# Seven products of half blocks in place of eight, in three blocks of a fused attention and expert kernel

## The chip, the cores and the metric

The kernel runs as one program on one core of a Trainium2 chip. The metric is the device time of one execution in microseconds (us). Lower is better.

## The reference

An attention with a pooled part and a local part gives x. A dense layer with an ELU in the middle works on x (this is layer 1), and a layer of four gated experts works on its result. All data are float32.

```python
# attention, 2 batches x 8 heads x 576 tokens x 64: pooled by 4, plus a band of +-3 tokens
x = attention(q, k, v)                      # 1152 tokens x 512
h = x @ w_in                                # 512 x 2048
g = np.where(h > 0.0, h, np.exp(np.minimum(h, 0.0)) - 1.0)
y = g @ w_out                               # 2048 x 512
for e in range(4):                          # p: normalised domain_probs
    out += p[:, e:e + 1] * (np.maximum(y @ w1[e], 0.0) @ w2[e])   # 512 x 1024 x 512
```

## The kernel before

**Splitting.** Every large product is made of three matmuls: an operand is split into a high part, which ScalarE casts, and a low part, which GpSimd (weights) or VectorE (activations) gets by a subtraction, and high by high, low by high and high by low are summed in PSUM. Each x, h, wa (up weights) and wb (down weights) thus exists as `_hi` and `_lo`.

**Layer 1** is cut into 8 blocks: 4 blocks of 512 hidden columns for the first batch of 576 tokens (blocks 0 to 3, mixed with the attention of the second batch) and the same 4 for the second batch (blocks 4 to 7). A block has 16 groups (`group1`), each of 12 matmuls of 128 x 128 by 288 tokens into one PSUM bank of 4 (`MOE_BANKS`). Groups 0 to 7 are the up projection (4 column tiles by 2 token halves), groups 8 to 15 the down projection. Behind an up group comes a chain: ScalarE takes relu(-h) (L782) and its exponential (L785), VectorE forms the ELU in PSUM (L1057), ScalarE casts `h_hi` (L791), VectorE subtracts `h_lo` (L1063). Behind a down group VectorE copies (block 4, L1078) or adds (L1080) the bank into `y_acc`, and its semaphore `y_added` frees the bank.

**Layer 2** is cut into 16 steps (`step2`): 8 halves of 512 hidden columns (two of each expert), each for the tokens of step 0 (2 x 256) and of step 1 (2 x 320). Its up projection is a two by two block product in Strassen's form (Winograd's variant): 7 products instead of 8. For this the weights need three sums of quarters (`s_raw`, L1343 to L1348 on GpSimd, then `s_hi` on ScalarE, L822, and `s_lo` on GpSimd, L1352), the tokens three sums of quarters (`add_y`: step 0 on GpSimd, L1316 to L1324, step 1 on VectorE, L1161 to L1169), and VectorE adds products to one another (`u2_sum` L1102, `w_sum` L1108, C22 L1114, C12 L1120, C21 L1125).

**Order.** It is written out by hand: each engine runs its own list, and semaphores tie them. The lists that matter are in `block`'s functions: `group1` on every engine, on GpSimd the sequence behind its loop (`split_wb`, `add_y(0)`, `split_wa`, `split_y(0)`, a memset of `o_acc` in block 5), on VectorE the four gate instructions ahead of block 5 (L1254 to L1260). SyncE loads wa and wb of the next block when both parts of the present one exist.

Of the kernel before, what the change touches and what calls it, by code (L numbers as in the profile page):

```python
# [54 lines left out]

QF = FB // 2
# [8 lines left out]
T2_, T1_, T4_ = range(3)  # L65
# [36 lines left out]
def program(nc, q, k, v, w_in, w_out, probs, w1, w2, out):  # L102
# [12 lines left out]
    with ExitStack() as ctx:  # L115
# [110 lines left out]
        t_raw_ready = sem("t_raw_ready")  # L226
        qT_copied, kT_copied = sem("qT_copied"), sem("kT_copied")
# [123 lines left out]
        def _(pe):  # L351
# [202 lines left out]

            def step2(j, b):
# [27 lines left out]

                pe.wait_ge(y_lo_ready, Y_PARTS * b + 2)
# [5 lines left out]
                pe.wait_ge(s_lo_ready, 3 * j + 1)  # L590
# [14 lines left out]
                for p in range(PAIRS2):  # L605
                    pe.wait_ge(u2_ready, PAIRS2 * v + p + 1)
                    product2(bank(BANK_B, p), weights(1, 0, p), tokens(0, 1), False, False, p7_done)
                pe.wait_ge(s_lo_ready, 3 * j + 3)
                for p in range(PAIRS2):
                    pe.wait_ge(w_ready, PAIRS2 * v + p + 1)  # L610
                    product2(bank(BANK_C, p), weight_sum(S4, p), tokens(1, 1), False, True, p3_done)
                pe.wait_ge(y_lo_ready, Y_PARTS * b + 7)
                for p in range(PAIRS2):
                    pe.wait_ge(c22_ready, PAIRS2 * v + p + 1)
# [97 lines left out]
            with pe.Fori(BLOCKS1 + 1, 2 * BLOCKS1) as w:  # L712
                for g in range(GROUPS1):
                    group1(w, 1, g)
# [8 lines left out]
        def _(act):  # L723
# [83 lines left out]
            def split_first2(n):  # L807

                act.wait_ge(wa_loaded, 16 * (2 * BLOCKS1 + 1))
                act.wait_ge(group_done, groups_before1(2 * BLOCKS1 - 1) + UP1)  # L810
                split_w2(0, n)

            def split_w2(j, n):

                if n in (0, 1, 3, 4):
                    c = n if n < 2 else n - 1
                    act.wait_ge(s_raw_ready, 4 * j + 3)
                    nc.scalar.copy(wa_hi[:, c, :], wa_raw[:, c, :]).then_inc(wa_hi_ready, 1)  # L818
                else:
                    q = {2: S2, 5: S1, 6: S4}[n]  # L820
                    act.wait_ge(s_raw_ready, 4 * j + 4 if q == S4 else 4 * j + 3)
                    nc.scalar.copy(s_hi[:, q], s_raw[:, q]).then_inc(s_hi_ready, 1)  # L822

            def step2(j, b, border=False):
# [19 lines left out]
                for p in range(PAIRS2):  # L844
                    act.wait_ge(p2_done, PAIRS2 * v + p + 1)
# [6 lines left out]
                for p in range(PAIRS2):  # L852
                    act.wait_ge(c22_ready, PAIRS2 * v + p + 1)
# [6 lines left out]
                for p in range(PAIRS2):  # L860
                    act.wait_ge(c12_ready, PAIRS2 * v + p + 1)
                    hidden_hi(0, 1, p, BANK_C)
                for p in range(PAIRS2):
                    act.wait_ge(c21_ready, UNIT_CREDIT + PAIRS2 * v + p + 1)
                    hidden_hi(1, 0, p, BANK_B)

            def next_weights2(j):

                act.wait_ge(p4_done, PAIRS2 * (2 * j + 2))
                act.wait_ge(wa_loaded, 16 * (2 * BLOCKS1 + j + 2))  # L870
                for n in range(KC + 3):
                    split_w2(j + 1, n)
# [87 lines left out]
            after = {9 + n: [(split_y, 0, n)] for n in range(Y_PARTS)}  # L960
            for g in range(GROUPS1):
                group1(BLOCKS1, 1, g, after.get(g, ()))
            with act.Fori(BLOCKS1 + 1, 2 * BLOCKS1 - 1) as w:
                for g in range(GROUPS1):
                    group1(w, 1, g)
# [496 lines left out]
```

## Time and profile before

| what | value |
|---|---|
| three runs | 659.1, 659.1, 659.29 us |
| median | 659.1 us |
| profiled execution, its own time | 658.5 us |
| span in its trace, first to last instruction | 656.7 us |
| mean granted TensorE clock | 0.999 |

The span leaves 1.8 us of the profiled execution's time ahead of and behind the instructions. The profiled execution is 0.6 us shorter than the median of the runs.

### The profile page before, as it was taken

What the parts mean: (1) busy time and instruction counts of PE and PEld (TensorE: products, weight loads), DVE (VectorE), ACT (ScalarE), POOL (GpSimd) and SP (SyncE); (2) the same over time, 40 slices, a digit from 0 to 9 for tenths busy, and PEclk for the clock granted to TensorE, in tenths of its full rate; (3) what the DMA queues carried; (4) which work ended last, traced back from release to release, by engine and by line L of the source; (5) the groups of instructions that cost most, each with busy time, mean ns of one, the idle gap of its engine ahead of it and who ended that gap; (6) DMA issues with size and microseconds to landing.
All of it is one profiled execution on the core that took longest, in us unless ns stands there. A gap on an engine that the chain in (4) does not pass through costs nothing.

```text
span 656.7 us, 12912 instructions
## 1 busy us (share of the span) xinstructions
PE 647.1 (99%) x4734; PEld 597.4 (91%) x4734; DVE 321.6 (49%) x715; ACT 278.3 (42%) x759; POOL 304.5 (46%) x266
## 2 busy tenths in 40 slices
PE   8999999999999999999999999999999999999998
PEld 5788999999999999998998998899899899899986
DVE  5856454545354343475534544453464355265352
ACT  4888383838295374464224133142152152142110
POOL 4674444443399444888426336138047065160210
PEclk9999999999999999999999999999999999999999
DMA  9954434332112311301103003003011011010012
GB/s 184 246 131 110 122 83 117 87 94 73 64 65 67 127 64 64 117 12 65 65 1 129 1 0 128 0 6 122 0 64 64 0 64 64 1 64 1 1 49 96
DMA packets 51489, 46.11 MB, mean 70 GB/s; under 512 B 31616, under 2 KB 33920, under 8 KB 51456
## 3 DMA queue, kind: packets, MB, share of 16 engines
q1 hardware_dynamic: 51456, 45.67, 23.5%
q8 instruction: 21, 0.34, 0.2%
q14 instruction: 12, 0.10, 0.0%
HBM read 43.30 MB, written 2.36 MB: 70 GB/s over the span
## 4 chain that ended last, share of the span: by engine, by line
PE 90%; ACT 5%; DVE 4%; issue 1%; ACTq 0%; DVEq 0%
PE psum L474 19%; PE psum L476 19%; PE psum L475 19%; PE psum L549 9%; PE psum L551 9%; PE psum L547 9%; ACT attn L741 1%; PE psum L466 1%; DVE neg_max L1013 1%; ACT attn_p L741 1%; PE psum L397 1%; PE psum L460 1%; PE psum L421 1%; ACT sums L782 1%; PE psum L441 1%
## 5 line engine op out<-in xcount | busy, mean ns | idle before, releaser
L1302 POOL TENSOR_TENSOR wb_lo<-wb_raw,wb_hi 128x512 fp32r<-128x512 f32 x64 | 82.0, 1295 | 202.4 <-ACT wb_hi L774 202.4
L1142 DVE SCALAR_TENSOR_TENSOR o_acc<-psum,gate_now,o_acc 128x512 f32<-128x512 f32 x72 | 54.1, 751 | 126.0 <-PE psum L476 125.7
L476 PE MATMUL psum<-wb_hi,h_lo 128*128 128x512 f32 x288 | 112.3, 390 | 0.0
L475 PE MATMUL psum<-wb_lo,h_hi 128*128 128x512 f32 x288 | 112.2, 390 | 0.0
L474 PE MATMUL psum<-wb_hi,h_hi 128*128 128x512 f32 x288 | 112.0, 389 | 0.0
L831 ACT ACTIVATE h_hi<-psum 128x320 fp32r<-128x320 f32 (+1 forms) x128 | 52.5, 412 | 87.4 <-DVE psum L1114 40.4
L1302 POOL TENSOR_TENSOR wa_lo<-wa_raw,wa_hi 128x512 fp32r<-128x512 f32 x60 | 76.0, 1294 | 22.6 <-ACT wa_hi L818 14.1
L837 ACT COPY sums<-psum 128x256 f32<-128x256 f32 (+1 forms) x32 | 12.8, 400 | 156.7 <-PE psum L551 156.7
L474 PE MATMUL psum<-h_hi,wb_hi 128*128 128x288 f32 x256 | 76.8, 300 | 0.0
L476 PE MATMUL psum<-h_hi,wb_lo 128*128 128x288 f32 x256 | 75.4, 294 | 0.0
L475 PE MATMUL psum<-h_lo,wb_hi 128*128 128x288 f32 x256 | 75.3, 294 | 0.0
L474 PE MATMUL psum<-x_hi,wa_hi 128*128 128x288 f32 x232 | 70.0, 302 | 1.7 <-DVE h_lo L1063 1.2
L475 PE MATMUL psum<-x_lo,wa_hi 128*128 128x288 f32 x232 | 68.3, 295 | 0.0
L476 PE MATMUL psum<-x_hi,wa_lo 128*128 128x288 f32 x232 | 68.3, 295 | 0.0
L476 PEld LDWEIGHTS psum<-wb_hi,h_lo 128*128 128x128 f32 x288 | 54.0, 188 | 11.3
L474 PEld LDWEIGHTS psum<-wb_hi,h_hi 128*128 128x128 f32 x288 | 54.1, 188 | 10.8
L475 PEld LDWEIGHTS psum<-wb_lo,h_hi 128*128 128x128 f32 x288 | 54.0, 188 | 10.8
L1096 DVE SCALAR_TENSOR_TENSOR h_lo<-psum,h_hi 128x320 fp32r<-128x320 f32 (+1 forms) x128 | 54.9, 450 | 17.0 <-ACT h_hi L831 17.0
L551 PE MATMUL psum<-x_hi,wa_lo 128*128 128x256 f32 (+1 forms) x192 | 56.8, 296 | 0.0
L549 PE MATMUL psum<-x_lo,wa_hi 128*128 128x256 f32 (+1 forms) x192 | 56.7, 295 | 0.0
L547 PE MATMUL psum<-x_hi,wa_hi 128*128 128x256 f32 (+1 forms) x192 | 56.6, 295 | 0.0
L1057 DVE SCALAR_TENSOR_TENSOR psum<-sums,psum 128x288 f32<-128x288 f32 x64 | 29.6, 462 | 45.9 <-ACT sums L785 45.9
(163 smaller groups left out, 1529.0 us busy)
## 6 DMA issues: line engine op xcount, KB each, us to landing
wa_raw<-in_moe_w_in SPq DMA_DIRECT2D x8, 1024.0 KB, 5.7
wb_raw<-in_moe_w_out SPq DMA_DIRECT2D x8, 1024.0 KB, 5.0
wa_raw<-in_moe_w SPq DMA_DIRECT2D x8, 1024.0 KB, 4.9
wb_raw<-in_moe_w SPq DMA_DIRECT2D x8, 1024.0 KB, 5.0
out<-o_acc SPq DMA_DIRECT2D x9, 256.0 KB, 2.0
q_in<-in_q SPq DMA_DIRECT2D x10, 144.0 KB, 4.3
k_in<-in_k SPq DMA_DIRECT2D x10, 144.0 KB, 4.3
v_in<-in_v SPq DMA_DIRECT2D x5, 288.0 KB
```

The lines of the kernel that those rows point to most:

```text
L474: nc.tensor.matmul(bank_cols, w_hi(n), x_hi_(n), start=(n == 0), stop=False)
L475: nc.tensor.matmul(bank_cols, w_hi(n), x_lo_(n), start=False, stop=False)
L476: last = nc.tensor.matmul(bank_cols, w_lo(n), x_hi_(n), start=False, stop=(n == chunks - 1))
L547: nc.tensor.matmul(bank, w_op[0][:, k, :], x_op[0][:, k, :], start=(start and k == 0), stop=False, skip_group_check=True)
L549: nc.tensor.matmul(bank, w_op[0][:, k, :], x_op[1][:, k, :], start=False, stop=False, skip_group_check=True)
L551: last = nc.tensor.matmul(bank, w_op[1][:, k, :], x_op[0][:, k, :], start=False, stop=(stop and k == 1), skip_group_check=True)
L741: last = nc.scalar.activation(out[:, c, :], psum[:, bank, width * (c - c0):width * (c - c0 + 1)], ACT.Exp, bias=neg_max[:, stat:stat + 1], ...
L831: nc.scalar.activation(h_hi[:, 2 * fh + p, t0 + width * th:t0 + width * (th + 1)], psum[:, bank[p], 0:width], ACT.Relu).then_inc(h_hi_read ...
L1057: nc.vector.scalar_tensor_tensor(bank, elu_exp[:, g % 2, 0:N1], -1.0, bank, ALU.add, ALU.max).then_inc(elu_ready, 1)
L1096: nc.vector.scalar_tensor_tensor(h_lo[at], bank(banks, p), 0.0, h_hi[at].bitcast(F32), ALU.max, ALU.subtract).then_inc(h_lo_ready, 1)
L1142: nc.vector.scalar_tensor_tensor(o_acc[:, m, :], psum[:, DOWN2_BANKS[(MT * half + m) % 2], :], gate_now[:, m:m + 1], o_acc[:, m, :], ALU.m ...
L1302: nc.gpsimd.tensor_tensor(lo[:, c, :], raw[:, c, :], hi[:, c, :].bitcast(F32), ALU.subtract).then_inc(lo_ready, 1)
```

## The change

Block 4 stays in the old form. Blocks 5, 6 and 7 (`block7`, `BLOCKS7 = 3`, `FIRST7 = 5`) form their up projection of 512 columns by 576 tokens from seven products of half blocks, with 288 tokens a half, in the way of `step2`. Their down projection keeps its 96 matmuls, in another order: the four groups of the first token half first take hidden chunks 0 and 1, then 2 and 3; the other four follow whole. It uses banks 6, 7, 0, 3, 6, 7, 6, 7.

TensorE's list of the up projection and the two gates that the down projection has at its end:

```diff
+            def block7(w):
+                for p in range(PAIRS2):
+                    pe.wait_ge(y_added, y_before - 5 + p)
+                    product2(bank(BANK_A, p), weights(0, 0, p), tokens(0, 0), True, False, p1_done)
+                pe.wait_ge(s_lo_ready, 3 * v + 1)
+                for p in range(PAIRS2):
+                    product2(bank(BANK_B, p), weight_sum(S2, p), token_sum(T2_), True, False, p6_done)
...
+                    product2(bank(BANK_A, p), weights(0, 1, p), tokens(1, 0), False, True, p2_done)
...
+                    product2(bank(BANK_C, p), weight_sum(S1, p), token_sum(T1_), True, False, p5_done)
...
+                    pe.wait_ge(u2_ready, PAIRS2 * v + p + 1)
+                    product2(bank(BANK_B, p), weights(1, 0, p), tokens(0, 1), False, False, p7_done)
+                for p in range(PAIRS2):
+                    pe.wait_ge(c22_ready, PAIRS2 * v + p + 1)
+                    product2(bank(BANK_B, p), weights(1, 1, p), token_sum(T4_), False, True, p4_done)
...
+                    product2(bank(BANK_C, p), weight_sum(S4, p), tokens(1, 1), False, True, p3_done)
...
+                pe.wait_ge(h_lo_ready, h_before + 8)
+                for g in range(KC, 2 * KC):
+                    pe.wait_ge(y_added, y_before + (1, 2, 5, 6)[g - KC])
+                    for f in range(FC):
+                        down(g, f)
```

The sums of x quarters need x unsplit. The attention of the second batch therefore writes its output into the second half of `y_acc` (free until block 4's down projection) and not into `x_sum`, and VectorE forms four sums ahead of block 4's groups; T3 takes the place of the x quarter (0, 1).

```diff
+            def add_x():
+                dve.wait_ge(out_free, OUT_CREDIT + 2 * PAIRS)
+                nc.vector.tensor_tensor(xt_raw(T1_), x_quad(0, 1), x_quad(0, 0), ALU.subtract).then_inc(xt_raw_ready, 1)
+                nc.vector.tensor_tensor(xt_raw(T3_), x_quad(1, 1), x_quad(0, 1), ALU.subtract).then_inc(xt_raw_ready, 1)
...
+            add_x()
+            lows = {12: [(xt_lo, 1, T2_)], 13: [(xt_lo, 2, T1_)], 14: [(xt_lo, 3, T4_)], 15: [(xt_lo, 4, T3_)]}
```

VectorE runs something beside the `y_acc` adds of each new block (`beside(g)` behind the add of group g): in block 5 the token sums of step 0 (`add_y(0, g)`, before on GpSimd), in block 6 the gates, in block 7 the memset of `o_acc` (before on GpSimd), whose first three rows serve as `s_raw1` until then.

```diff
+                for g in range(2 * KC):
+                    dve.wait_ge(group_done, groups_before7(w) + g + 1)
+                    nc.vector.tensor_tensor(y_acc[at], psum[:, DOWN7_BANKS[g], 0:N1], y_acc[at], ALU.add).then_inc(y_added, 1)
+                    beside(g)
...
+            def clear_out(g):
+                if g == 0:
+                    dve.wait_ge(s_lo_ready, 3 * BLOCKS7)
+                    nc.vector.memset(o_acc[:], 0.0).then_inc(acc_zeroed, 1)
```

GpSimd's list behind its loop:

```diff
-            add_y(0)
-            split_wa(BLOCKS1 + 1)
-            split_y(0)
-            split_wb(BLOCKS1 + 1)
-            nc.gpsimd.memset(o_acc[:], 0.0).then_inc(acc_zeroed, 1)
...
+            add_ws(FIRST7, s_raw1)
+            split_ws(FIRST7, s_raw1)
+            split_wb(FIRST7)
+            pool.wait_ge(s_lo_ready, 3)
+            add_ws(FIRST7 + 1, s_raw1)
+            split_ws(FIRST7 + 1, s_raw1)
+            split_y(0, range(3))
+            split_wb(FIRST7 + 1)
...
+            split_ws(FIRST7 + 2, s_raw1)
+            split_y(0, range(3, Y_PARTS))
```

ScalarE copies the first product twice a block (`copy_p1`), has the same ELU chain with a buffer of its own (`elu7`), and casts the next block's weights and weight sums at the block's end (`split_ws`).

How the lists stand, at three places. VectorE at the end of block 5, before:

```order
L1063 TENSOR_TENSOR h_lo<-psum,h_hi 128x288 [waits h_hi_ready] x2
L1076 ISA
L1080 TENSOR_TENSOR y_acc<-psum,y_acc 128x288 [waits group_done]
L1076 REGISTER_ALU
L1080 TENSOR_TENSOR y_acc<-psum,y_acc 128x288 [waits group_done]
```

and in the changed kernel (L1299 is `h_lo`, L1356 the add into `y_acc`, `h_spare` the memory of the token sums):

```order
L1299 TENSOR_TENSOR h_lo<-psum,h_hi 128x288 [waits h_hi_ready] x2
L1356 TENSOR_TENSOR y_acc<-psum,y_acc 128x288 [waits group_done]
L1436 TENSOR_TENSOR h_spare<-y_acc 128x512 [waits y_added]
L1356 TENSOR_TENSOR y_acc<-psum,y_acc 128x288 [waits group_done]
L1440 TENSOR_TENSOR y_acc<-y_acc 128x2x256 [waits t_raw_ready]
L1356 TENSOR_TENSOR y_acc<-psum,y_acc 128x288 [waits group_done]
L1443 TENSOR_TENSOR h_spare<-y_acc,h_spare 128x512
L1356 TENSOR_TENSOR y_acc<-psum,y_acc 128x288 [waits group_done]
```

Between the first five adds of block 5 now stand four operations of 512 elements. At the end of block 7, VectorE in the changed kernel:

```order
L1299 TENSOR_TENSOR h_lo<-psum,h_hi 128x288 [waits h_hi_ready] x2
L1356 TENSOR_TENSOR y_acc<-psum,y_acc 128x288 [waits group_done]
L1559 MEMSET o_acc 128x4608 [waits s_lo_ready]
L1356 TENSOR_TENSOR y_acc<-psum,y_acc 128x288 [waits group_done] x7
```

The memset stands between the first add and the other seven; before, it was GpSimd's (L1422), in block 5. TensorE in the middle of a new block (the first matmul of each product; L571 is `product2`'s first line):

```order
L571 MATMUL psum<-x_hi,wa_hi 128x288 [waits u2_ready]
...
L571 MATMUL psum<-t_hi,wa_hi 128x288 [waits c22_ready]
L573 MATMUL psum<-t_lo,wa_hi 128x288
L575 MATMUL psum<-t_hi,wa_lo 128x288
```

The first row opens the second half of product 7, and the row with `c22_ready` the first half of product 4, which follows at once. In `step2` product 3 lies between the two.

## Rows read from the trace of the kernel before

**Rows 1.** the page: busy time of TensorE with its share.

```profile
PE 647.1 (99%) x4734; PEld 597.4 (91%) x4734; DVE 321.6 (49%) x715; ACT 278.3 (42%) x759; POOL 304.5 (46%) x266
```

**Rows 2.** waits of TensorE: us in total, times, longest.

```profile
PE psum L474 <- DVE h_lo L1063: 1.2, 1, 1.2
```

**Rows 3.** TensorE's timeline (start us, us, line): block 5, two steps of layer 2.

```profile
202.45 0.29 PE L474 MATMUL psum<-x_hi,wa_hi 128*128 128x288 f32 x1
...
278.77 0.28 PE L547 MATMUL psum<-x_hi,wa_hi 128*128 128x256 f32 x1
...
288.73 0.30 PE L547 MATMUL psum<-x_hi,wa_hi 128*128 128x320 f32 x1
```

**Rows 4.** timeline of VectorE in block 6: two adds into y_acc.

```profile
250.33 0.46 DVE L1080 TENSOR_TENSOR y_acc<-psum,y_acc 128x288 f32<-128x288 f32 x1 [1.14 <-PE psum L476]
251.93 0.46 DVE L1080 TENSOR_TENSOR y_acc<-psum,y_acc 128x288 f32<-128x288 f32 x1 [1.14 <-PE psum L476]
```

**Rows 5.** timeline around a wait of TensorE in block 0.

```profile
57.43 0.46 DVE L1063 TENSOR_TENSOR h_lo<-psum,h_hi 128x288 fp32r<-128x288 f32 x1 [1.39 <-ACT h_hi L791]
57.95 0.41 PE L474 MATMUL psum<-x_hi,wa_hi 128*128 128x288 f32 x1 [1.24 <-DVE h_lo L1063]
58.19 0.30 PE L475 MATMUL psum<-x_lo,wa_hi 128*128 128x288 f32 x1
```

**Rows 6.** timeline: last matmul of a product 7 in step2, C22 behind it.

```profile
285.06 0.28 PE L551 MATMUL psum<-x_hi,wa_lo 128*128 128x256 f32 x1
...
285.38 0.43 DVE L1114 TENSOR_TENSOR psum<-psum,sums 128x256 f32<-128x256 f32 x1 [0.28 <-PE psum L551]
```

**Rows 7.** timeline of the ELU chain and the casts in block 7.

```profile
263.05 0.41 ACT L782 ACTIVATE sums<-psum 128x288 f32<-128x288 f32 x1 [0.40 <-PE psum L476]
263.97 0.46 DVE L1057 SCALAR_TENSOR_TENSOR psum<-sums,psum 128x288 f32<-128x288 f32 x1 [0.75 <-ACT sums L785]
...
267.17 0.46 DVE L1057 SCALAR_TENSOR_TENSOR psum<-sums,psum 128x288 f32<-128x288 f32 x1 [0.77 <-ACT sums L785]
267.54 1.02 DVE L1063 TENSOR_TENSOR h_lo<-psum,h_hi 128x288 fp32r<-128x288 f32 x2
267.67 0.40 ACT L791 CAST h_hi<-psum 128x288 fp32r<-128x288 f32 x1 [0.24 <-DVE psum L1057]
267.96 1.14 ACT L818 CAST wa_hi<-wa_raw 128x512 fp32r<-128x512 f32 x2
```

**Rows 8.** timeline of GpSimd (POOL) at the border to layer 2.

```profile
268.66 2.56 POOL L1302 TENSOR_TENSOR wa_lo<-wa_raw,wa_hi 128x512 fp32r<-128x512 f32 x2 [0.81 <-ACT wa_hi L818]
```

**Rows 9.** timeline: VectorE and GpSimd at the same time, at three places.

```profile
33.01 0.72 POOL L1292 TENSOR_TENSOR v_sum<-v_sum,v_part 72x256 f32<-72x256 f32 x1
33.38 1.83 DVE L1050 TENSOR_TENSOR x_lo<-x_sum,x_hi 128x576 fp32r<-128x576 f32 x1
33.69 0.90 POOL L1297 TENSOR_TENSOR attn_p<-attn_p,recip 128x432 f32<-128x432 f32 x1
...
110.24 0.74 POOL L1288 TENSOR_TENSOR v_sum<-v_in 72x256 f32<-72x256 f32 x1 [8.13 <-DMA v_in<-in_v]
110.25 1.34 DVE L1050 TENSOR_TENSOR x_lo<-x_sum,x_hi 128x576 f32 x1
...
202.33 2.57 POOL L1332 TENSOR_TENSOR x_lo<-y_acc,x_hi 128x512 fp32r<-128x512 f32 x2
203.97 0.99 DVE L1260 TENSOR_TENSOR gate<-gate,gate_sum 128x36 f32<-128x36 f32 x1
```

**Rows 10.** groups of VectorE by form: memsets (us in total, mean ns).

```profile
L1172 DVE MEMSET zeros<- 128x256 uint32 x1 | 0.3, 272 | 0.9 <-PEq L1452 0.9
L1178 DVE MEMSET qTs<- 128x16 f32 x1 | 0.1, 72 | 0.1
```

**Rows 11.** timeline of VectorE at the start of block 4.

```profile
177.42 0.76 DVE L1050 TENSOR_TENSOR x_lo<-x_sum,x_hi 128x576 f32 x1
180.54 0.46 DVE L1057 SCALAR_TENSOR_TENSOR psum<-sums,psum 128x288 f32<-128x288 f32 x1 [2.36 <-ACT sums L785]
```

More of the change, by code:

```diff
@@ L64 @@
 S2, S1, S4 = range(3)
-T2_, T1_, T4_ = range(3)
+T2_, T1_, T4_, T3_ = range(4)
 T_RAW = (0, 1, 3)
@@ L582, in bank_free @@
                     pe.wait_ge(h_lo_ready, UPS_LAYER1 + TILES_STEP * (v - 1) + PAIRS2 * place + p + 1)
+                if isinstance(j, int) and v == 0:
+                    pe.wait_ge(y_added, Y_CREDIT + T1 * KC * BLOCKS1 * BATCH - 4)
                 pe.wait_ge(y_lo_ready, Y_PARTS * b + 2)
@@ L711, in _ @@
                 group1(BLOCKS1, 1, g)
-            with pe.Fori(BLOCKS1 + 1, 2 * BLOCKS1) as w:
-                for g in range(GROUPS1):
-                    group1(w, 1, g)
+            with pe.Fori(FIRST7, 2 * BLOCKS1) as w:
+                block7(w)
             step2(0, 0)
@@ L959, in _ @@
                 mixed_block1(i, i + HALF_PAIRS)
[L960 to L965, printed above, removed]
-            after = {UP1 + 1 + n: [(split_first2, n)] for n in range(KC + 3)}
-            for g in range(GROUPS1):
-                group1(2 * BLOCKS1 - 1, 1, g, after.get(g, ()), False)
+            for g in range(UP1 + 1):
+                group1(BLOCKS1, 1, g, next_wa=False)
+            split_ws(FIRST7, 0)
+            split_ws(FIRST7, 1)
+            split_ws(FIRST7, 2)
+            xt_hi(T2_)
+            split_ws(FIRST7, 3)
+            split_ws(FIRST7, 4)
+            xt_hi(T1_)
+            split_ws(FIRST7, 5)
+            split_ws(FIRST7, 6)
+            xt_hi(T4_)
+            xt_hi(T3_)
+            block7(FIRST7)
+            for n in range(3):
+                split_y(0, n)
+            block7(FIRST7 + 1)
+            for n in range(3, Y_PARTS):
+                split_y(0, n)
+            block7(FIRST7 + 2)
             step2(0, 0, True)
@@ new lines, in _, with gates @@
+            block7(FIRST7, token_sums)
+            def gates(n):
+                if n == 0:
+                    dve.wait_ge(probs_loaded, 16)
+                    nc.vector.tensor_reduce(gate_sum[:], gate[:], X, ALU.add).then_inc(gate_step, 1)
+                elif n == 1:
+                    dve.wait_ge(gate_step, 1)
+                    nc.vector.tensor_scalar(gate_sum[:], gate_sum[:], EPS, None, ALU.add).then_inc(gate_step, 1)
+                elif n == 2:
+                    dve.wait_ge(gate_step, 2)
+                    nc.vector.reciprocal(gate_sum[:], gate_sum[:]).then_inc(gate_step, 1)
+                elif n == 3:
+                    dve.wait_ge(gate_step, 3)
+                    nc.vector.tensor_tensor(gate[:], gate[:], gate_sum[:].unsqueeze(2).to_broadcast([128, MT, EXPERTS]),
+                                            ALU.mult).then_inc(gate_step, 1)
@@ L1262, in _ @@
+            block7(FIRST7 + 1, gates)
+            def clear_out(g):
+                if g == 0:
+                    dve.wait_ge(s_lo_ready, 3 * BLOCKS7)
+                    nc.vector.memset(o_acc[:], 0.0).then_inc(acc_zeroed, 1)
+            block7(FIRST7 + 2, clear_out)
             dve.wait_ge(gate_step, 4)
-            with dve.Fori(BLOCKS1 + 1, 2 * BLOCKS1) as w:
-                for g in range(GROUPS1):
-                    group1(w, 1, g)
-            add_y(1)
+            for n in range(4):
+                add_y(1, n)
```

390 lines of the change are left out of this document (285 added, 105 removed).

## The prediction

> **What bounds the kernel now.** First the page: TensorE is busy for 99% of the span and no other engine for more than half [rows 1]. Then its waits: there is one of over 1.2 us in 656.7 us [rows 2], in block 0. Then the blocks in question: block 5 starts at 202.45 and the first step of layer 2 at 278.77 [rows 3], so blocks 5 to 7 take 76.32 us, 25.44 us each, with no gap. A matmul less is thus time gained, and a wait that TensorE has not had before is time lost in full. The questions are how many matmuls go, and whether the lists around them keep up.
>
> **Matmuls.** An up projection falls from 96 to 84 matmuls of 288 columns. In the down projection a group of 12 takes 1.60 us, 0.1333 us each [rows 4], so its 96 take 12.80 us, and the 96 of the up projection the other 12.64 us, 0.1317 each. Layer 2 has the same seven products: 84 matmuls of 256 columns in 9.96 us, 0.1186 each, without a gap [rows 3]. I take 0.1325 for a product's matmul at 288 columns (between 0.1317 and 0.1333). The new block is 84 x 0.1325 = 11.13, plus 12.80, so 23.93 us. Gain: 25.44 - 23.93 = 1.51 us a block, 4.53 us for three. Bounds from the two pitches: 4.3 to 4.7.
>
> **The new chain inside a block.** I count from the block's first matmul. A pair of half products takes 1.59 us: P1 at 0, P6 at 1.59, P2 3.18, P5 4.77, P7 6.36, P4 7.95, P3 9.54, down projection 11.13. VectorE sees a product 0.32 us after the start of its last matmul [rows 6]. P4's first half needs C22, which VectorE forms behind P7's first half (seen at 7.35). But VectorE is late there by its queue. P2's halves are seen at 4.16 and 4.96. From relu to ELU it is 0.92 us, from ELU to cast 0.50, and queued operations follow at 0.37 [rows 7]. First ELU 5.09; `w_sum` 0 at 5.76 when P5 is seen; second ELU 6.13; `h_lo` 0 at 6.50, `w_sum` 1 6.87, `h_lo` 1 7.24 (its cast began at 6.63 and is done), C22 at 7.61, with 0.46 done at 8.07. TensorE starts 0.06 us after a releaser's end, and its next matmul then comes 0.24 behind instead of 0.13 [rows 5]: P4 starts at 8.13 instead of 7.95 and loses 0.11 more, 0.29 us a block, 0.9 us for three. Bounds: 0 if the queue is one place (0.37) shorter, 0.6 if as much longer. The second half of P4 has 0.4 us to spare. The other waits in this part are met: `u2_sum` is done at 3.1 for P7 at 6.36, `w_sum` at 7.3 for P3.
>
> Four more ELU chains alternate between ScalarE and VectorE. By the same pitches the last cast starts at 14.8, the last `h_lo` at 15.25 and is done at 15.7. The second half of the down projection asks for it at 17.8 (11.42 + 48 x 0.1333), so 2 us of cover; the four groups before ask for chunks 2 and 3 at 14.6 and 15.0 and have them at 13.0 and 14.1. Cost nothing; with 2 us more in the chain it would begin to show.
>
> **Block 5, token sums on VectorE.** The add of group 0 starts at 15.62. Behind each of the first four adds now stands an operation of 512 elements with both inputs in SBUF. GpSimd works then: ScalarE casts the next block's weights from 15.10 (0.29 after the last `h_hi`), GpSimd starts 0.70 after the cast's start, so 15.75 to 15.80, and goes through seven operations of 1.28 us one behind the other [rows 7, 8]. The trace shows what happens when both want this. `x_lo` at 110.25 took 1.34 us beside a GpSimd operation that ended at 110.98, and the gate product of 36 elements took 0.99 us, to the end of GpSimd's at 204.90 [rows 9]: VectorE waits for the end of the running operation, and its own work is then 0.6 us. The adds into `y_acc`, with one input in PSUM, stay at 0.46 us beside a busy GpSimd. So the first sum waits until 17.0 and ends at 17.6; then each add and sum take a GpSimd operation and a sum's own 0.57, 1.82 us together: sums end at 17.6, 19.4, 21.2, 23.0. The add of group 4 starts at 22.95, is done at 23.4, and TensorE's group 6 needs its bank at 21.02 (`y_added` + 5). It starts at 23.5, and with the restart that is **2.6 us lost**. Lower bound 0 (GpSimd gives way, sums of 0.6 us: add 4 by 20.3). Upper bound: `x_lo` at 33.38 took 1.83 us, over the end of one GpSimd operation and the whole of the next [rows 9]; if each sum waits for two, add 4 is done at 28.4 and 7.6 us are lost. I take the first, since two of the three places show it.
>
> The Trainium skill ("SBUF — State Buffer", section "Who interferes with whom") says that VectorE operations with two SBUF inputs and GpSimd's reads exclude one another for a whole instruction and that the first to issue has the port. By that rule it is one operation waited for and 2.6 us; the row at 33.38 speaks for more, and by it the loss would be 7.6.
>
> **Block 6, gates.** Two of the four small operations wait in the same way, up to 1.3 us each, but the add of group 4 can start at 19.62 at the earliest and finds VectorE free then. Nothing.
>
> **Block 7, memset on VectorE.** It stands behind the add of group 0 and starts at 16.0. The trace has 256 elements in 272 ns, 1.06 ns each [rows 10]; 4608 take 4.9 us. The slope between the two memset rows (72 ns for 16) gives 0.83 ns and 3.9 us. Queued behind it is the add of group 1, which starts at 20.8 and is done at 21.3. TensorE's group 5 needs that bank at 19.42 (`y_added` + 2). It starts at 21.3: with the restart **2.0 us lost** (1.0 by the shorter one). The later adds catch up before group 6 asks. I take 4.9, since it is the nearer row in size.
>
> The Trainium skill ("VectorE: DVE Perf Modes", section "Zero memsets can be issued as uint32 (trn2)") has one cycle per element, which at 0.96 GHz would be an estimate of 4.8 us; the sum would be lower by 0.1.
>
> **Block 4, sums of x.** Four operations of 576 elements, 0.76 us each, 0.7 apart, go between `x_lo` at 177.42 and the first ELU at 180.54 [rows 11]. VectorE is idle there for 2.36 us and GpSimd too; the ELU moves from 180.5 to about 181.1, and its cast has to wait on ScalarE anyway. Nothing, at most 0.3. The low parts of these sums, in the last four groups, wait for GpSimd as above, but their adds have four banks and the first reader comes 1.6 us into block 5.
>
> **GpSimd's list.** A new block has 15 operations of 1.28, 19.2 us of 23.9 (before: 8). Token splits add three in block 6 and four in block 7. Counted on: `wb_lo` of block 7 is complete 10.5 us into it, and the down projection asks at 11.4. 0.9 us of cover, nothing lost, and nothing gained when the memset and the sums leave GpSimd, since nobody waited for them. SyncE's loads keep their order and have over 5 us.
>
> **Sum.** -4.5 + 0.9 + 2.6 + 2.0 = +1.0 us (+0.94 unrounded). On the profiled execution: span 657.6, own time 659.4. It was 0.6 us under the median of the three runs, so the median should be **660.0 us**. A measurement can tell about 0.2%, 1.3 us: this is no change.
>
> **Rivals.**
> 1. GpSimd gives way. VectorE's sums go through in 0.6 us and block 5 loses nothing: 660.0 - 2.6 = 657.4. For it: a sum that issues just ahead of a GpSimd operation goes first. Against: GpSimd's seven follow without a gap. 0.18.
> 2. Neither place in VectorE's queue is felt, because the groups come later than I count or the port is free: 659.1 - 4.5 + 0.9 = 655.5. 0.10.
> 3. Slower: VectorE loses the port twice per sum in block 5, as at 33.38. 7.6 instead of 2.6: 665.0; with half the sums so, 662.5. It decides where a second GpSimd operation slips in. 0.14.
> 4. GpSimd late in block 7: at 1.35 us an operation the 25 between the casts of block 6 and this point take 1.8 us more, the cover of 0.9 is gone, TensorE waits for `wb_lo` 0.9 us or more: 661 to 661.5. 0.10.
> 5. The memset runs at twice the speed (2.4 us) and costs nothing: 658.0. 0.08.
>
> **How the numbers follow.** The forecast has 0.40, with a range of its own of 658.9 to 660.9 (memset 1.0 to 2.0, C22 0 to 0.6 a block). Faster by over 0.2% (below 657.8) is rivals 1 and 2 with a little of 5: 0.30. Within: three quarters of the forecast and most of 5: 0.38. Slower (above 660.4): the rest of the forecast, rivals 3 and 4: 0.32. The range of 8 in 10 leaves out rival 2 and the upper half of rival 3: 656.0 to 663.5.
>
> **What the changed profile would show.** Blocks 5, 6, 7 of 26.8, 24.2 and 26.2 us. If the first half of P4 starts without a gap, the chain step is wrong. In block 5, sums of 1.6 us on VectorE and one wait of TensorE for `y_acc` (L1356) of 2.5 us; sums of 0.6 say rival 1, of 2.9 rival 3. In block 7, a memset of 4.9 us and a wait of 1.9; a row of 2.4 says rival 5. A wait of TensorE for `wb_lo` says rival 4. The prediction is wrong altogether if `product2` runs at another pitch at 288 columns, or if TensorE waits at the start of a block.

## The result, and the profile after

| what | before | changed kernel |
|---|---|---|
| median of 18 runs each, on one chip | 659.19 us | 660.22 us |
| lowest and highest | 658.56, 659.52 | 659.57, 660.96 |
| ratio of the changed kernel to before, 95% interval | | 1.0015 [1.0008, 1.0022] |
| profiled execution, its own time | 658.5 us | 660.32 us |
| span in its trace | 656.7 us | 658.5 us |
| mean granted TensorE clock | 0.999 | 0.997 |
| TensorE's first matmul of block 4, at | 176.66 us | 176.90 us |
| of block 5, at | 202.45 us | 202.70 us |
| of the first step of layer 2, at | 278.77 us | 280.60 us |
| length of blocks 5 to 7 | 76.32 us | 77.90 us |

The time was forecast at 660.0 us and is 660.22. The change makes the kernel slower by 0.15% (0.08 to 0.22% by the interval): 1.03 us between the medians, 0.9 by the forecast. Blocks 5 to 7 took 1.58 us more. Another 0.24 us of the 1.8 us between the two spans lie ahead of block 4, in the attention stage: the start of block 4 differs from one execution to the next (176.66 to 177.69 in the thirteen traces of this study, the kernel before among them). So lengths of blocks 5 to 7 are compared below rather than spans. From the first step of layer 2 to the end the two spans are the same, 377.93 and 377.90 us.

The page of the changed kernel, busy time with the share of the span (it answers to [rows 1]):

```profile
PE 645.4 (98%) x4698; PEld 594.3 (90%) x4698; DVE 346.1 (53%) x758; ACT 286.8 (44%) x778; POOL 323.9 (49%) x282
```

36 matmuls fewer, 12 for each new block. At 0.1325 us each they are 4.8 us, but TensorE's busy time fell by 1.7 us only. Part of the gain seems to have gone to matmuls that took longer or started further apart, before any wait is counted. The waits of TensorE (us in total, times, longest), against [rows 2]:

```profile
PE psum L641 <- DVE y_acc L1356: 3.6, 2, 1.9
```

These are the two waits of the forecast, one in block 5 and one in block 7. The blocks on TensorE's timeline of the changed kernel (start us, us, line), against [rows 3]:

```profile
202.70 0.29 PE L571 MATMUL psum<-x_hi,wa_hi 128*128 128x288 f32 x1
...
230.45 0.29 PE L571 MATMUL psum<-x_hi,wa_hi 128*128 128x288 f32 x1
...
254.55 0.29 PE L571 MATMUL psum<-x_hi,wa_hi 128*128 128x288 f32 x1
...
280.60 0.28 PE L571 MATMUL psum<-x_hi,wa_hi 128*128 128x256 f32 x1
```

Blocks 5, 6 and 7 take 27.75, 24.10 and 26.05 us, where 26.8, 24.2 and 26.2 were forecast. Blocks 6 and 7 are right to 0.15 us, block 5 is 0.95 us longer. The same three blocks as stretches of the trace (stretch, us, then busy us and instructions of PE, PEld, DVE, ACT, POOL, then TensorE's granted clock, DMA share, GB/s):

```profile
202.70:230.45 27.75, 25.86 (x183) 25.40 (x181) 19.86 (x40) 16.98 (x40) 22.30 (x17) 0.94 0.23 80
230.45:254.55 24.10, 24.10 (x183) 23.87 (x181) 15.40 (x38) 17.30 (x41) 20.71 (x17) 1.00 0.17 61
254.55:280.60 26.05, 24.35 (x182) 23.89 (x181) 17.43 (x35) 15.22 (x37) 24.14 (x20) 1.00 0.31 106
```

The same matmuls keep TensorE busy for 25.86 us in block 5 and for 24.10 us in block 6, and the granted clock of block 5 is 0.94. The third column from the end tells of a cost that no wait shows.

**Block 5, the wait.** VectorE at its down projection:

```profile
218.59 1.53 DVE L1436 TENSOR_TENSOR h_spare<-y_acc 128x512 f32<-128x512 f32 x1
220.05 0.45 DVE L1356 TENSOR_TENSOR y_acc<-psum,y_acc 128x288 f32<-128x288 f32 x1
220.41 1.42 DVE L1440 TENSOR_TENSOR y_acc<-y_acc 128x512 f32<-128x512 f32 x1
...
223.82 1.39 DVE L1447 TENSOR_TENSOR h_spare<-y_acc,h_spare 128x512 f32<-128x512 f32 x1
225.14 0.81 DVE L1356 TENSOR_TENSOR y_acc<-psum,y_acc 128x288 f32<-128x288 f32 x2
```

GpSimd beside them:

```profile
218.28 3.00 POOL L1600 TENSOR_TENSOR wa_lo<-wa_raw,wa_hi 128x512 fp32r<-128x512 f32 x2 [3.31 <-ACT wa_hi L931]
...
222.94 3.42 POOL L1600 TENSOR_TENSOR wa_lo<-wa_raw,wa_hi 128x512 fp32r<-128x512 f32 x2
```

The four token sums take 1.39 to 1.53 us each, the adds with PSUM between them 0.45 us beside the same busy GpSimd. The add of group 4 starts at 225.14, which is 22.44 us into the block (forecast 22.95).

**Block 5, the clock.** TensorE behind that add:

```profile
225.64 0.40 PE L641 MATMUL psum<-h_hi,wb_hi 128*128 128x288 f32 x1 [1.89 <-DVE y_acc L1356]
...
226.14 0.44 PE L641 MATMUL psum<-h_hi,wb_hi 128*128 128x288 f32 x1
226.38 0.44 PE L642 MATMUL psum<-h_lo,wb_hi 128*128 128x288 f32 x1
...
229.50 0.31 PE L643 MATMUL psum<-h_hi,wb_lo 128*128 128x288 f32 x1
229.65 0.29 PE L641 MATMUL psum<-h_hi,wb_hi 128*128 128x288 f32 x1
```

From 226.14 to 229.50 matmuls start 0.24 us apart and are 0.44 us long; behind that they are 0.133 apart and 0.29 long again. Three stretches of the trace show the granted clock (columns as above), the third in block 6:

```profile
226.00:228.00 2.00, 2.00 (x11) 2.00 (x10) 0.00 (x0) 0.00 (x0) 2.00 (x3) 0.53 0.25 18
228.00:229.00 1.00, 1.00 (x6) 1.00 (x5) 0.46 (x1) 0.00 (x0) 1.00 (x2) 0.50 0.64 217
...
231.00:232.00 1.00, 1.00 (x10) 1.00 (x9) 0.11 (x1) 0.56 (x2) 1.00 (x2) 1.00 0.04 12
```

That is the lower of the clock's two levels, 1.2 GHz in place of 2.4, for about 3.4 us. Ahead of it TensorE had stood still for 1.89 us and had then started three matmuls at the full clock.

**Block 7, the memset.** VectorE, and TensorE behind it:

```profile
271.44 3.90 DVE L1559 MEMSET o_acc<- 128x4608 f32 x1 [0.91 <-issue]
275.25 1.49 DVE L1356 TENSOR_TENSOR y_acc<-psum,y_acc 128x288 f32<-128x288 f32 x4
...
275.70 0.40 PE L641 MATMUL psum<-h_hi,wb_hi 128*128 128x288 f32 x1 [1.70 <-DVE y_acc L1356]
```

TensorE's matmul ahead of this started at 273.71 and would have been followed at 273.84 without a wait, so this gate costs 1.86 us and the slower restart 0.11 (next matmul at 275.94), 1.97 together. By the block's length, against block 6, it is 1.95.

**Inside a block, C22.** VectorE's row that forms both halves of C22, and TensorE at the step from product 7 to product 4:

```profile
210.27 1.02 DVE L1315 TENSOR_TENSOR psum<-psum,sums 128x288 f32<-128x288 f32 x2
...
210.49 0.29 PE L575 MATMUL psum<-x_hi,wa_lo 128*128 128x288 f32 x1
...
210.78 0.40 PE L571 MATMUL psum<-t_hi,wa_hi 128*128 128x288 f32 x1
211.01 0.29 PE L573 MATMUL psum<-t_lo,wa_hi 128*128 128x288 f32 x1
```

C22 starts 7.57 us into the block (forecast 7.61), and the two spacings of 0.29 and 0.23 in place of 0.133 cost 0.26 us a block (forecast 0.29).

So 76.32 us became 77.90 in this way: 4.80 less for the matmuls (three blocks of 23.84 in place of 25.44), 0.78 more for C22, 2.15 for block 5's wait with its restart (2.17 by the rows: 223.45 to 225.64 in place of 0.133, and 0.11), 1.50 for the lower clock (14 spacings of 0.24 in place of 0.133) and 1.95 for block 7's wait.

### The profile page after: what moved, and what is told of

Read it like the earlier page. It is cut to its first block, busy times and chain, and to the rows that moved or that the text cites. A ratio compares the mean times of both kernels' runs of the same rounds, so it can differ in the third digit from the quotient of the medians.

```text
span 658.5 us, 12934 instructions
## 1 busy us (share of the span) xinstructions
PE 645.4 (98%) x4698; PEld 594.3 (90%) x4698; DVE 346.1 (53%) x758; ACT 286.8 (44%) x778; POOL 323.9 (49%) x282
## 4 chain that ended last, share of the span: by engine, by line
PE 86%; SPq 4%; ACT 4%; DVE 3%; DMA 1%; issue 1%; POOL 0%; ACTq 0%; POOLq 0%
PE psum L498 15%; PE psum L500 15%; PE psum L499 15%; PE psum L571 11%; PE psum L573 11%; PE psum L575 11%; SPq L297 2%; PE psum L641 2%; PE psum L643 2%; PE psum L642 2%; DMA k_in<-in_k 1%; SPq L308 1%; SPq L305 1%; ACT attn L856 1%; PE psum L490 1%
## 5 line engine op out<-in xcount | busy, mean ns | idle before, releaser
L575 PE MATMUL psum<-x_hi,wa_lo 128*128 128x256 f32 (+2 forms) x228 | 67.4, 296 | 0.0
L571 PE MATMUL psum<-x_hi,wa_hi 128*128 128x256 f32 (+2 forms) x228 | 67.3, 295 | 0.0
L573 PE MATMUL psum<-x_lo,wa_hi 128*128 128x256 f32 (+2 forms) x228 | 67.3, 295 | 0.0
L498 PE MATMUL psum<-h_hi,wb_hi 128*128 128x288 f32 x160 | 48.5, 303 | 0.0
L500 PE MATMUL psum<-h_hi,wb_lo 128*128 128x288 f32 x160 | 47.1, 295 | 0.0
L499 PE MATMUL psum<-h_lo,wb_hi 128*128 128x288 f32 x160 | 47.1, 295 | 0.0
L573 PE MATMUL psum<-t_lo,s_hi 128*128 128x320 f32 (+2 forms) x152 | 44.9, 296 | 0.0
L571 PE MATMUL psum<-t_hi,s_hi 128*128 128x320 f32 (+2 forms) x152 | 44.8, 295 | 0.0
L575 PE MATMUL psum<-t_hi,s_lo 128*128 128x320 f32 (+2 forms) x152 | 44.8, 295 | 0.0
L571 PEld LDWEIGHTS psum<-x_hi,wa_hi 128*128 128x128 f32 x228 | 43.1, 189 | 0.6
```

The source lines that it names most:

```text
L498: nc.tensor.matmul(bank_cols, w_hi(n), x_hi_(n), start=(n == 0), stop=False)
L499: nc.tensor.matmul(bank_cols, w_hi(n), x_lo_(n), start=False, stop=False)
L500: last = nc.tensor.matmul(bank_cols, w_lo(n), x_hi_(n), start=False, stop=(n == chunks - 1))
L571: nc.tensor.matmul(bank, w_op[0][:, k, :], x_op[0][:, k, :], start=(start and k == 0), stop=False, skip_group_check=True)
L573: nc.tensor.matmul(bank, w_op[0][:, k, :], x_op[1][:, k, :], start=False, stop=False, skip_group_check=True)
L575: last = nc.tensor.matmul(bank, w_op[1][:, k, :], x_op[0][:, k, :], start=False, stop=(stop and k == 1), skip_group_check=True)
```

## Experiments

Two things had to be told apart. The first is what the waits are made of: my theory is that VectorE's token sums wait for GpSimd's operations and that the memset fills VectorE for 4.8 us; the rivals are that the sums are slow by themselves (their layout, or the memory they go to), and that TensorE waits for something else that merely ends at the same time. The second came only with the profile: the slow matmuls behind the wait in block 5. Theory: the granted clock falls because TensorE stood still, so it goes when the wait is made short; rival: it belongs to this place in the program (the loads and ScalarE's casts at the end of block 5) or to chance, and stays.

The experiments that change two or more things combine the edits of the single ones. Blocks 5 to 7 below are always from TensorE's first matmul of block 5 to its first of layer 2.

**e1: the token sums of step 0 on GpSimd again**, behind its split of `wb_lo` for block 4. The last sum of the four is shown.

```diff
-            block7(FIRST7, token_sums)
+            block7(FIRST7, lambda g: None)
...
             split_wb(BLOCKS1)
+            pool_add_y()
...
+                nc.gpsimd.tensor_tensor(t_raw(0, T4_), y_quad(0, 1, 0), t_raw(0, T2_), ALU.subtract
+                                        ).then_inc(t_raw_ready, 1)
```

> Undoes one part: the four token sums of step 0 go back to GpSimd, ahead of the weight sums of block 5, where GpSimd has 5 us to spare; VectorE has only the adds in block 5. Theory (VectorE's sums lock with GpSimd's splits, TensorE waits 1.9 us for the add of group 4, and its clock then falls to half for 3.3 us): both go, block 5 takes 24.2 us instead of 27.75, and the time is 660.2 - 3.5 = 656.7. Rival (the clock falls at this place whatever TensorE waits for): block 5 takes 25.7, the time is 658.3. Rival (GpSimd's list is too full, its weight sums come late for block 5): waits for wa_lo or s_lo take the place of those for y_acc, no gain or a loss.

Measured: 657.74 us (7 runs) against 659.54 for the kernel before, ratio 0.9970 [0.9959, 0.9981]. Blocks 24.39, 24.10, 26.06, together 74.55 us, which is 3.35 less than the changed kernel. TensorE's waits:

```profile
PE psum L641 <- DVE y_acc L1356: 1.7, 1, 1.7
```

One wait is left, block 7's. The wait and the slow matmuls of block 5 left together. The 3.35 us are the 2.15 of the wait and the 1.50 of the clock, less a new loss of 0.29: product 2 of block 5 waits for the low part of its weights, which GpSimd finishes late. That costs 0.19 us and a slower restart of 0.10. The time is 1 us above what was expected for it, of which 0.76 goes with the start of block 4, at 177.66 in the traced execution.

**e2: the memset in six pieces**, three of 1024 elements in block 6 and three of 512 behind the adds of groups 3 to 5 of block 7.

```diff
             def gates(n):
+                if 3 < n < 7:
+                    nc.vector.memset(o_acc[:, 2 * n - 5:2 * n - 3, :], 0.0).then_inc(acc_zeroed, 1)
...
-                if g == 0:
+                if g == 3:
                     dve.wait_ge(s_lo_ready, 3 * BLOCKS7)
-                    nc.vector.memset(o_acc[:], 0.0).then_inc(acc_zeroed, 1)
+                if 3 <= g < 6:
+                    nc.vector.memset(o_acc[:, g - 3, :], 0.0).then_inc(acc_zeroed, 1)
...
-            dve.wait_ge(acc_zeroed, 1)
+            dve.wait_ge(acc_zeroed, 6)
```

> Changes one part: the memset of o_acc is six pieces, three of 1024 elements behind the adds of groups 4 to 6 of block 6 and three of 512 behind groups 3 to 5 of block 7, instead of one of 4608 behind group 0 of block 7. Theory (the add of group 1 stands behind 4.8 us of memset): TensorE's wait of 1.7 us in block 7 goes, with its restart 1.85; block 7 takes 24.2 instead of 26.05; time 658.4. Rival (that wait is made by the late start of the memset, 0.9 us of issue, or by something else in the queue): at least 0.9 us of it stays, 659.3 or more.

Measured: 658.27 us (12 runs), ratio 0.9981 [0.9972, 0.9990]. Blocks 27.78, 24.09, 24.09, together 75.96. Only block 7 changed, by 1.96 us, and TensorE's remaining wait is block 5's:

```profile
PE psum L641 <- DVE y_acc L1356: 1.9, 1, 1.9
```

**e3: the wait in block 5 made longer**, by a memset of 1280 elements of scratch behind the fourth sum.

```diff
                     add_y(0, g)
+                if g == 3:
+                    nc.vector.memset(sums2[:, 1:3], 0.0)
```

> Adds a memset of 1280 elements on VectorE (1.3 us, of buffers that are dead there) behind the fourth token sum, so that TensorE's wait in block 5 grows from 1.9 to 3.2 us. If a wait costs what it lasts: 660.2 + 1.3 = 661.5. If the fall of the clock hangs on the wait's length, and the changed kernel is at its edge (6 of its 18 runs show a mean clock of 1.000 and 659.6, 12 show 0.997 and 660.3): all runs show 0.997 or less, and the time is 661.6 or more. The clock's rows around the wait are the point.

Measured: 661.80 us (6 runs), ratio 1.0038 [1.0026, 1.0050]. Block 5 is 28.94 us, 1.19 more. The wait grew from 1.9 to 3.2 us:

```profile
PE psum L641 <- DVE y_acc L1356: 4.9, 2, 3.2
```

The add of group 4 comes 23.78 us into the block, 1.34 later than in the changed kernel, TensorE's gap is 1.28 longer, from start to start, and the block 1.19. The clock around the end of the wait (columns as above; the next matmul starts at 227.32):

```profile
225.00:227.10 2.10, 0.00 (x0) 0.00 (x0) 1.88 (x3) 0.00 (x0) 2.10 (x3) 1.00 0.00 0
227.10:230.50 3.40, 3.17 (x13) 3.18 (x14) 0.53 (x2) 0.00 (x0) 3.40 (x4) 0.50 0.65 208
```

The slow stretch is no longer than in the changed kernel, and 0.2 us of it lie in the wait, where they cost nothing; the rest of the longer wait is paid in full. All 6 executions have a mean granted clock of 0.997.

**e4: the changed kernel as it is**, on the chip and beside the runs of e1 to e3.

> The changed kernel once more, for a second trace of it beside the others on the same chip. Time 660.2, some runs at 659.6 with a mean clock of 1.000. If this trace is one of those, block 5 shows no half clock, and what it loses in its place (0.8 of the 1.5 us that the half clock costs must be somewhere) can be seen.

Measured: 660.64 us (12 runs), ratio 1.0016 [1.0007, 1.0025]; blocks 5 to 7 take 77.90 us again, and two of its 12 executions have a mean clock of 1.0. These two took 659.66 and 659.67 us, the ten others 660.24 to 661.22. The 18 runs of the result fall apart in the same way: six at 1.0 of 659.57 to 659.61 us, twelve at 0.997 of 660.14 to 660.96.

**e5: GpSimd held** during block 5's token sums. A wait for the fifth add is put ahead of the next low part of the weight sums. Two groups of token splits move behind `split_wb`, so that the weights are in time; the first is shown.

```diff
             add_ws(FIRST7 + 1, s_raw1)
+            pool.wait_ge(y_added, Y_CREDIT + T1 * KC * FIRST7 + 5)
             split_ws(FIRST7 + 1, s_raw1)
-            split_y(0, range(3))
             split_wb(FIRST7 + 1)
+            split_y(0, range(3))
...
```

> The changed kernel with GpSimd held back: it starts the seven splits in block 5 only behind VectorE's fifth add (the splits of the step 0 tokens go behind those of wb to make up for it). The token sums stay on VectorE. Theory (the sums took 1.4 us because GpSimd held the path both share): they take 0.65 us each, TensorE's wait of 1.9 us in block 5 goes and with it the half clock; blocks 5 to 7 take 77.9 - 3.5 = 74.4 us, time 656.7, plus what a later GpSimd may cost in blocks 6 and 7 (up to 1). Rival (the sums are slow on VectorE for another reason, such as their strided access): 1.4 us each and the wait of 1.9 us stay, 660.2 or more.

Measured: 657.76 us (8 runs) against 659.59, ratio 0.9973 [0.9962, 0.9984]. Block 5 takes 24.10 us, like block 6. Two of the four sums on VectorE, and what GpSimd does there:

```profile
218.39 0.68 DVE L1436 TENSOR_TENSOR h_spare<-y_acc 128x512 f32<-128x512 f32 x1
...
220.32 0.68 DVE L1443 TENSOR_TENSOR h_spare<-y_acc,h_spare 128x512 f32<-128x512 f32 x1
...
222.52 2.54 POOL L1600 TENSOR_TENSOR wa_lo<-wa_raw,wa_hi 128x512 fp32r<-128x512 f32 x2 [7.75 <-DVE y_acc L1356]
```

The same instructions on the same memory take 0.68 us with GpSimd idle and 1.39 to 1.53 us with GpSimd at work. That shows the theory of the first question and excludes that the sums are slow by themselves. The Trainium skill ("SBUF — State Buffer", section "Who interferes with whom") says that such operations of VectorE and GpSimd's reads shut one another out for whole instructions; these two traces agree.

**e6: the wait in block 5 made shorter**, by moving the fourth sum behind the add of group 4.

```diff
-                if g < 4:
+                if g < 3:
                     add_y(0, g)
+                if g == 4:
+                    add_y(0, 3)
```

> The fourth token sum moves behind the add of group 4, so that TensorE's wait in block 5 shrinks from 1.9 to about 0.5 us. If the clock's fall hangs on this wait, no run shows it: blocks 5 to 7 take 77.9 - 1.4 - 1.5 = 75.0 us, and the time is 657.3. If the fall comes from the place and not from the wait: the clock still falls behind it, 658.8.

Measured: 658.25 us (11 runs), ratio 0.9979 [0.9970, 0.9988]. Blocks 24.95, 24.09, 26.06, together 75.10. TensorE's gap in block 5 is 0.87 us from start to start. The sums before it are as slow as ever:

```profile
218.54 1.52 DVE L1436 TENSOR_TENSOR h_spare<-y_acc 128x512 f32<-128x512 f32 x1
```

This one separates wait and clock. In the changed kernel the gap is 2.19 us, so the wait shrank by 1.32, but block 5 is 2.80 us shorter. The remaining 1.48 us are the slow stretch, which is gone. None of the 11 executions shows the lower clock; of the changed kernel's 32 executions 23 do, so this is not chance. Loads and casts at this place are those of the changed kernel, so the rival that the place itself slows TensorE falls.

**e7: e1 and e2 together.**

> Both mends together: token sums of step 0 on GpSimd ahead of block 5, memset in six pieces. The two gains were 3.35 and 1.94 us in blocks 5 to 7. If they add: these blocks take 77.9 - 5.3 = 72.6 us, time 655.4 (0.6% under the kernel before). Rival (with the waits gone GpSimd's list is the limit and wb_lo of block 7 comes late): 73.5 or more.

Measured: 655.83 us (5 runs), ratio 0.9941 [0.9927, 0.9955]; blocks 24.39, 24.09, 24.09, together 72.57 us. The gains of e1 and e2 add up.

**e8: e7 and C22 one place earlier** in VectorE's queue, for its first half.

```diff
                 sum_w(1)
-                lo_part(1, 0, 0, BANK_A)
                 sum_c22(0)
+                lo_part(1, 0, 0, BANK_A)
                 sum_c22(1)
```

> As e7, and VectorE forms the first half of C22 ahead of the second h_lo of the block (one place earlier in its list). Theory (TensorE loses 0.26 us a block there, because C22 stands one place too far back): the gap before product 4 goes, 0.8 us less in three blocks, 71.8 us, time 654.6. Rival (C22 waits for product 7 itself, not for its place): the gap stays, 655.4.

Measured: 655.43 us (5 runs), ratio 0.9938 [0.9924, 0.9953]; blocks 24.27, 24.02, 24.02. The first half of product 4 now follows without a gap, but the expected 0.8 us came to 0.26. VectorE and TensorE in block 6 of this run:

```profile
234.07 0.47 DVE L1315 TENSOR_TENSOR psum<-psum,sums 128x288 f32<-128x288 f32 x1
234.44 0.45 DVE L1299 TENSOR_TENSOR h_lo<-psum,h_hi 128x288 fp32r<-128x288 f32 x1
235.03 0.47 DVE L1315 TENSOR_TENSOR psum<-psum,sums 128x288 f32<-128x288 f32 x1
...
234.54 0.29 PE L575 MATMUL psum<-x_hi,wa_lo 128*128 128x288 f32 x1
234.67 0.32 PE L571 MATMUL psum<-t_hi,wa_hi 128*128 128x288 f32 x1
...
235.36 0.30 PE L575 MATMUL psum<-t_hi,wa_lo 128*128 128x288 f32 x1
235.55 0.40 PE L571 MATMUL psum<-t_hi,wa_hi 128*128 128x288 f32 x1
```

C22's second half keeps its place in the list, but product 4 now asks for it 0.26 us sooner. It starts 8.28 us into the block (8.12 in e7), about when product 7's second half is finished, so here the rival (C22 waits for product 7 itself) is right. Spacings of 0.19 and 0.24 us in place of 0.133 stand at the start of product 4's second half: closing one gap uncovered the next. This is the fastest kernel of the study, 4.2 us under the kernel before beside it.

**e9: e5, e2 and e8's edit together**, so the token sums stay on VectorE with GpSimd held.

> The token sums stay on VectorE with GpSimd held back as in e5 (74.26 us for blocks 5 to 7 there), the memset is in pieces as in e2 and e7 (1.94 less), C22's first half is a place earlier as in e8 (0.08 a block less). If the three add: 72.1 us for blocks 5 to 7, and a time of 655.0 to 655.4, no better than e8 (72.31) by what a run can tell. Rival (with the memset gone from block 7 the held GpSimd comes too late with wb_lo there): 73 or more.

Measured: 657.13 us (5 runs) against 659.48, ratio 0.9965 [0.9952, 0.9979]. Blocks 5 to 7 take 72.00 us (24.00 each), as expected. The time does not follow: it is 1.7 to 2.1 us above what was expected. What TensorE waits for between 200 and 300 us, and VectorE at the start of layer 2:

```profile
PE psum L571 <- DVE sums L1376: 2.0, 1, 2.0
```

```profile
277.09 1.80 DVE L1440 TENSOR_TENSOR y_acc<-y_acc 128x640 f32<-128x640 f32 x1
...
280.76 2.06 DVE L1447 TENSOR_TENSOR h_spare<-y_acc,h_spare 128x640 f32<-128x640 f32 x1
```

The same sum (step 1's tokens) in the changed kernel:

```profile
282.22 0.82 DVE L1440 TENSOR_TENSOR y_acc<-y_acc 128x640 f32<-128x640 f32 x1
```

GpSimd in e9, and in e8, where the four sums stand between 275.55 and 278.82 and take 0.82 us each:

```profile
276.31 3.73 POOL L1644 TENSOR_TENSOR s_lo<-y_acc,s_hi 128x512 fp32r<-128x512 f32 x2
...
278.07 3.74 POOL L1629 TENSOR_TENSOR x_lo<-y_acc,x_hi 128x640 fp32r<-128x640 f32 x2 [2.95 <-ACT x_hi L1057]
```

e8 differs from e9 only in where the token sums of step 0 are formed and in e5's edit of GpSimd's list. There GpSimd is idle for 2.95 us at this point; in e9 it is behind with its splits and at work when VectorE forms the token sums of step 1. Three of these take 1.80 to 2.06 us in place of 0.82, the first product sum behind them is late, and TensorE waits 2.0 us. The collision that e5 took out of block 5 came back at the border. The clock does not fall behind this wait: it is 1.00 from 283 to 290 us in the trace, and the mean clocks of the 5 executions are 0.999 and 1.000.

**e10 and e11: the changed kernel twice more**, one execution each with its trace, for the clock.

> The changed kernel, one more look for a trace with a mean clock of 1.000. In such a trace block 5 should take 26.2 to 26.4 us (24.2 and the wait of 2 us) instead of 27.75 to 27.9, and block 5 should start about 0.8 us later than in the traces with 0.997, which makes 659.6.

> As e10_after_look: the changed kernel once more, same expectation.

Measured: e10 659.61 us, mean clock 1.000, blocks 26.25, 24.09 and 26.07; e11 660.90 us, mean clock 0.997, blocks 27.77, 24.10 and 26.06. The stretch behind the wait of block 5 in e10 (columns as above) has the full clock:

```profile
226.39:229.69 3.30, 3.30 (x24) 3.30 (x25) 0.77 (x2) 0.00 (x0) 3.30 (x4) 1.00 0.31 68
```

24 matmuls start within 3.3 us. In the changed kernel's first trace 14 spacings of 0.24 us took that long (226.14 to 229.50). The same kernel with the same wait has block 5 in 26.25 us at the full clock and in 27.75 at the lower one for a part: the clock costs 1.50 us. I had expected that a late start of this stage decides which it is. Block 4 starts at 177.65 in e10 and at 177.41 in e11, both late beside 176.90, and only e10 keeps its clock. A late start is thus not enough; that one later than 177.41 decides is not excluded, since the five traces with the lower clock start block 4 at 176.74 to 177.41.

The traces show one thing more. At the start of the kernel the granted clock is at its lower level and rises once: by the profile's record of the clock at 4.24 us in the changed kernel's first trace, at 5.55 in e11 and at 6.75 in e10. The same six small matmuls, in the first trace and in e10:

```profile
4.64 0.66 PE L386 MATMUL psum<-ident,q_in 96*128 96x96 f32 x6
...
5.03 1.17 PE L386 MATMUL psum<-ident,q_in 96*128 96x96 f32 x6
```

Block 4 starts late where that rise is late. And in all five traces with the lower clock in block 5 (the changed kernel, e2, e3, e4, e11) it falls 221.87 us behind the rise, 0.4 to 1.3 us after TensorE is back at work in four of them and 0.2 us before it in e3. The wait starts 218.4 to 219.2 us behind the rise in these five and 217.5 us in e10. So where the wait lies against that rise is a candidate for what decides, beside its length. No run moved this by itself.

## Why the prediction was right, and where it was not

| step, for blocks 5 to 7 | forecast | measured |
|---|---|---|
| matmuls at the full clock, a block | 23.93 | 23.84 (24.10 less 0.26 for C22) |
| C22 in time for product 4, a block | 0.29 | 0.26 |
| wait in block 5 | 2.6 | 2.15 |
| lower clock behind it | not foreseen | 1.50 |
| memset in block 7 | 2.0 | 1.95 |
| blocks 5 to 7 | 77.3 | 77.90 |

**Right.** The matmuls: 4.53 us were to be gained, and by 23.84 a block it is 4.8, a little above the upper bound of 4.7. C22: the place, the time (7.57 for 7.61) and the price came from counting VectorE's queue, and e8 shows that this queue is the cause for product 4's first half, since another order removes that gap. Block 6 gates nothing, the sums of x cost nothing (block 4 takes 25.80 us, the kernel before 25.79), and block 7's `wb_lo` was complete at 264.81, 10.26 us into the block (forecast 10.5, needed at 11.4), as GpSimd's row says:

```profile
259.77 5.04 POOL L1600 TENSOR_TENSOR wb_lo<-wb_raw,wb_hi 128x512 fp32r<-128x512 f32 x4
```

That excludes rival 4. Rivals 1, 2 and 5 (GpSimd gives way, no wait is felt, a fast memset) are excluded by the two waits. The memset: e2 returned 1.96 us for 2.0. I took 1.06 ns an element and 4.9 us. VectorE was occupied from 270.44 (the add ahead of it starts at 270.07, and queued operations follow at 0.37) to 275.25, 4.81 us. The lower bound of 3.9 us was a misreading: a row of a memset here does not show all that it occupies, as its 0.91 us of "issue" ahead of 3.90 us says, and so the slope between two such rows was too small.

**A term mis-sized.** The mechanism of block 5 is shown (e5, e1), its size was 2.6 for 2.15. The first add and its sum took 1.83 us, as forecast (1.82), the three others 1.70 each. With the first add 0.1 us earlier than counted, the add of group 4 started 22.44 instead of 22.95 us into the block. I had added a whole undisturbed GpSimd operation to a sum's own time, 0.1 us too much. At `x_lo`'s 1.83 us [rows 9] VectorE had lost the port twice; none of the four sums did here (rival 3).

**A step that was missing.** I priced a wait of TensorE by its length and the slower restart of [rows 5], and gave it no effect on the clock. In the changed kernel it has one: 1.50 us, in 23 of 32 executions. The mean granted clock tells the cases apart:

| TensorE's longest wait from block 5 on | kernels | executions at 0.997 |
|---|---|---|
| 3.2 us, in block 5 | e3 | 6 of 6 |
| 2.0 us, at the start of layer 2 | e9 | 0 of 5 |
| 1.9 us, in block 5 | the changed kernel, e2, e4, e10, e11 | 32 of 44 |
| 1.7 us, in block 7 | e1, e5, e6 | 0 of 26 |

The length of the wait alone does not order these rows.

The profile before could have raised the question, not answered it: it has no wait of over 1.2 us in a stage where TensorE is otherwise dense, and its clock is full.

**So the number was right in part by cancellation.** The missing 1.5 us of the clock stand against 0.36 us that matmuls and C22 came in lower, 0.45 of the wait and 0.05 of the memset: 77.90 for 77.3 (77.26 unrounded). In e10, the only execution of the changed kernel at the full clock that has a trace, blocks 5 to 7 took 76.41 us, 0.85 under the forecast and as long as in the kernel before. It still came out at 659.61 us, because its block 4 started 0.75 us later than in the first trace. The start of block 4 moves single executions by up to 1 us, as much as the whole effect. A smaller point: the forecast's own range began at 658.9, but with both of its lower bounds (memset 1.0, C22 0) the sum comes to 658.1.

**What stays open.** What decides whether the clock falls behind a wait of 1.9 us: not the place in the program alone (e6, e10) and not the length alone (e9). Where the wait lies against the clock's rise at the start of the kernel fits the six traces that have the wait in block 5, but only one of them (e10) keeps its clock, and it is not tested. Nor is it shown why the executions at the full clock lie so close together (659.57 to 659.67), or why single executions of the kernel before, beside e1 to e4, range from 658.49 to 661.11 us.

## What to carry to other kernels

Work that is moved to an idle engine costs what it costs beside its new neighbours: VectorE had time for the token sums by its busy share, but two inputs in SBUF beside a GpSimd without a gap made 0.68 us into 1.45, four times in front of the bank that TensorE waited for. Count the queue on the engine that frees the banks, place long operations where TensorE has banks to spare, and cut them (e2) rather than hold the other engine, because held work collides later (e9). Price a wait of TensorE of some 2 us with its length and with what the clock may take behind it, and look at the granted clock in the stretch behind every new wait.

## What the chip showed that was not expected

- A wait of 1.9 us in a dense stream of matmuls was followed by 3.4 us at the lower clock level in 32 of 44 executions, and one of 3.2 us in 6 of 6. Waits of 1.7 us, in 26 executions, and of 2.0 us at another place, in 5 (e9), were not. The longer wait cost no longer slow stretch (e3: 1.19 us more in all).
- The delay goes both ways: GpSimd is slowed by VectorE too. In e1, GpSimd's pair of splits beside VectorE's low parts of the x sums took 3.58 us, where such a pair takes 2.54 alone (e5):

```profile
203.09 3.58 POOL L1596 TENSOR_TENSOR wa_lo<-wa_raw,wa_hi 128x512 fp32r<-128x512 f32 x2
```

- A memset's row on VectorE is shorter than the time it fills: 3.90 us and 0.91 us of "issue" for 4608 elements. 4.8 us are 1.04 ns an element. The Trainium skill ("VectorE: DVE Perf Modes", section "Zero memsets can be issued as uint32 (trn2)") has one cycle an element for it. The estimate of 4.8 us that the prediction worked out from that agrees.
